# The rounded-off parts of four weight blocks made by an adding DMA and ScalarE instead of VectorE

## What is computed

```python
def _attn_ref(q, k, v, alpha):                 # per batch, head and step t
    state = alpha[t] * state + outer(k[t], v[t])
    y[t] = q[t] @ state
def _moe_ref(x, w_val, conv_w, w_out):
    gate = sigmoid(causal 5-tap convolution of x per feature)
    return (gate * (x @ w_val)) @ w_out
def _moe2_ref(x, w_ch1, w_ch2):
    u = x + real(fft(fft(x, axis=1), axis=2))
    un = (u - mean(u)) / np.sqrt(var(u) + 1e-06)
    return u + np.maximum(un @ w_ch1, 0.0) @ w_ch2
```

## Time and profile before

| | us |
|---|---|
| median of 3 runs | 550.87 |
| lowest, highest | 550.78, 551.3 |
| the profiled execution | 550.92 |
| its span in the trace | 548.8 |

### The profile page before, as it was taken

How to read it: one execution, slowest core, us unless ns; L and a number is a source line. 1 busy time by engine, 2 the same in 40 slices (tenths; PEclk the granted TensorE clock), 3 DMA queues, 4 the chain that set the end, 5 groups by cost and what they waited for, 6 DMA issues and landing times.

```text
span 548.8 us, 13477 instructions
## 1 busy us (share of the span) xinstructions
PE 540.8 (99%) x5547; PEld 519.5 (95%) x5547; DVE 400.5 (73%) x898; ACT 208.3 (38%) x487; POOL 13.0 (2%) x29
## 2 busy tenths in 40 slices
PE   7999999999999999999999999999999999999997
PEld 6988999999999999999999999999999999999997
DVE  7999899989858686989767486998936484653322
ACT  5565454425352135335262144325244133322221
POOL 0010000000000000000000000000000000000000
PEclk9999999999999999999999999999999999999999
DMA  8778202354312010455322001256300000022000
GB/s 255 237 265 301 67 25 63 112 159 133 82 47 81 30 33 26 136 145 175 93 62 68 29 1 45 85 142 191 83 4 27 30 2 0 1 59 83 11 23 30
DMA packets 36300, 47.20 MB, mean 86 GB/s; under 512 B 11632, under 2 KB 25200, under 8 KB 35984
## 3 DMA queue, kind: packets, MB, share of 16 engines
q1 hardware_dynamic: 34080, 40.97, 24.8%
q0 software_dynamic: 1728, 5.11, 2.6%
q10 hardware_dynamic: 432, 0.27, 0.2%
HBM read 35.32 MB, written 11.01 MB: 84 GB/s over the span
## 4 chain that ended last, share of the span: by engine, by line
PE 92%; DVE 4%; issue 1%; DMA 1%; ACT 1%; SPq 0%; DVEq 0%
PE bank L1062 45%; PE bank L1151 28%; PE evens L1089 4%; PE bank L1136 4%; PE bank L1131 2%; PE bank L1219 2%; PE bank L1182 2%; PE sums L1113 2%; PE bank L1253 1%; PE bank L1188 1%; DMA k_in<-in_k_dram 1%; DVE w_lo L985 1%; PE bank L1263 1%; PE sums L1098 0%; DVE scores L947 0%
## 5 line engine op out<-in xcount | busy, mean ns | idle before, releaser
L1044 DVE SCALAR_TENSOR_TENSOR h_lo<-bank,h_hi 128x256 fp32r<-128x256 f32 x144 | 60.2, 419 | 93.7 <-ACT h_hi L786 89.2
L1062 PE MATMUL bank<-unT_hi,w_hi 128*128 128x256 f32 x432 | 123.8, 286 | 1.0 <-DVE h_lo L1044 0.7
L786 ACT ACTIVATE h_hi<-bank 128x256 fp32r<-128x256 f32 x144 | 55.2, 383 | 177.0 <-PE bank L1062 176.9
L1062 PE MATMUL bank<-unT_lo,w_hi 128*128 128x256 f32 x432 | 122.1, 283 | 0.0
L1062 PE MATMUL bank<-unT_hi,w_lo 128*128 128x256 f32 x432 | 121.3, 281 | 0.0
L1151 PE MATMUL bank<-w_hi,h_hi 128*128 128x384 f32 x288 | 98.8, 343 | 0.0
L1151 PE MATMUL bank<-w_lo,h_hi 128*128 128x384 f32 x288 | 97.6, 339 | 0.0
L1151 PE MATMUL bank<-w_hi,h_lo 128*128 128x384 f32 x288 | 97.3, 338 | 0.0
L1062 PEld LDWEIGHTS bank<-unT_hi,w_hi 128*128 128x128 f32 x432 | 81.2, 188 | 4.3 <-DVE h_lo L1044 2.0
L1062 PEld LDWEIGHTS bank<-unT_hi,w_lo 128*128 128x128 f32 x432 | 81.6, 189 | 0.0
L1062 PEld LDWEIGHTS bank<-unT_lo,w_hi 128*128 128x128 f32 x432 | 81.4, 189 | 0.0
(11 more groups left out here) (192 smaller groups left out, 1016.5 us busy)
## 6 DMA issues: line engine op xcount, KB each, us to landing
v_in<-in_v_dram SPq DMA_DIRECT2D x24, 224.0 KB, 2.9
w_raw<-in_w_dram SPq DMA_DIRECT2D x2, 2304.0 KB, 10.3
a_in<-in_alpha_dram SPq DMA_DIRECT2D x44, 96.9 KB, 2.3
q_in<-in_q_dram SPq DMA_DIRECT2D x44, 96.0 KB, 2.2
k_in<-in_k_dram SPq DMA_DIRECT2D x44, 96.0 KB, 2.3
turned_blocks<-turned SPq DMA_DIRECT2D x15, 256.0 KB, 2.2
kdT<-turned_blocks SPq DMA_DIRECT2D x60, 64.0 KB, 2.0
out_dram<-u POOLq DMA_DIRECT2D x18, 192.0 KB, 2.4
```

The source lines that it names most:

```text
L786: act.activation(h_hi[:, f % HBUF, :], ps[:, 0:GW], ACT.Relu).then_inc(s_hi, 1)
L1044: dve.scalar_tensor_tensor(h_lo[:, f % HBUF, :], ps[:, 0:GW], 0.0, h_hi[:, f % HBUF, :].bitcast(F32), ALU.max, ALU.subtract).then_inc(s_re ...
L1062: last = pe.matmul(ps, l, r, start=(i == 0), stop=(i == len(mms) - 1))
```

## The change

Pieces 1 and 2 of `w1` and `w2` (four blocks) are prepared another way; piece 0 and all other tables are not touched. For each of the four blocks:

1. ACT's `whi` writes minus the rounded weights (scale -1) to the place of the high part.
2. POOL waits for it and issues a DMA from that place to the raw weights, with addition (`accum_op`): in the raw weights' bytes now stands raw minus high. It moves 128 x 1536 elements of 4 bytes, 768 KB, from SBUF to SBUF. A semaphore of its own tells its end.
3. ACT's new form of `wlo` waits for that semaphore and writes the sum onto itself, rounded to fp32r. DVE's subtraction is gone.
4. ACT's new step `wpos` multiplies the high part by -1 in place. PE waits for this step (`weights_hi_positive`) instead of DVE's.

The steps are placed anew: `whi` of both pieces 1 moves from the MLP's slots 0 and 1 to the front, right behind `whi` of `w2`'s piece 0; the new `wlo` of `w1` piece 1 stands at the front's end, ahead of the steps `t`; the others are listed in `FIRST`.

```diff
@@ front(b)
-        sch += [("wlo", 0, WN.index("w1"), 0)] + attention(n, 0, "inv") + [("whi", 0, WN.index("w2"), 0)]
+        sch += [("wlo", 0, WN.index("w1"), 0)] + attention(n, 0, "inv") + [("whi", 0, WN.index("w2"), 0), ("whi", 0, WN.index("w1"), 1), ("whi", 0, WN.index("w2"), 1)]
...
-        sch += attention(n, 0, "scale")
+        sch += attention(n, 0, "scale") + [("wlo", 0, WN.index("w1"), 1)]
@@ FIRST
-         "wlo": ((1, 1, "w1"), (2, 1, "w2"), (6, 2, "w1"), (7, 2, "w2")), "x": (15, 26), "gate": (25, 36),
+         "wlo": ((0, "wpos", "w1", 1), (1, "wlo", "w2", 1), (2, "wpos", "w2", 1), (2, "whi", "w1", 2), (3, "whi", "w2", 2), (6, "wlo", "w1", 2), (6, "wpos", "w1", 2), (7, "wlo", "w2", 2), (8, "wpos", "w2", 2)), "x": (15, 26), "gate": (25, 36),
@@ GpSimd
+                if kind == "whi" and by_dma(a, f):
+                    pool.wait_ge(s_whi, WHI_AT[w] + 1)
+                    raw, negative = (part(w_[WN[a]], a, f) for w_ in (w_raw, w_hi))
+                    pool.dma_start(raw, negative.bitcast(F32), accum_op=ALU.add).then_inc(s_wadd[WADD_AT[("wlo",) + w[1:]]], 16)
@@ ScalarE
-                    act.activation(high, raw, ACT.Copy, scale=0.5 if WN[a] == "wout" else 1.0).then_inc(s_whi, 1)
+                    scale = 0.5 if WN[a] == "wout" else -1.0 if by_dma(a, f) else 1.0
+                    act.activation(high, raw, ACT.Copy, scale=scale).then_inc(s_whi, 1)
+                elif kind == "wlo" and by_dma(a, f):
+                    act.wait_ge(s_wadd[WADD_AT[w]], 16)
+                    high, low, sums_ = (part(w_[WN[a]], a, f) for w_ in (w_hi, w_lo, w_raw))
+                    act.activation(low, sums_, ACT.Copy)
+                elif kind == "wpos":
+                    high = part(w_hi[WN[a]], a, f)
+                    act.activation(high, high.bitcast(F32), ACT.Copy, scale=-1.0).then_inc(s_wpos, 1)
@@ VectorE
-                elif kind == "wlo":
+                elif kind == "wlo" and not by_dma(a, f):
@@ TensorE
-                pe.wait_ge(s_wlo, WLO_AT["wlo", 0, WN.index(name), j] + 1)
+                w = ("wlo", 0, WN.index(name), j)
+                if w in WADD_AT:
+                    pe.wait_ge(s_wpos, WADD_AT[w] + 1)
+                else:
+                    pe.wait_ge(s_wlo, WLO_AT[w] + 1)
```

More of the change, by code:

```diff
@@ L108, in front @@
     if b == 0:
-        sch += [("wlo", 0, WN.index("w1"), 0)] + attention(n, 0, "inv") + [("whi", 0, WN.index("w2"), 0)]
+        sch += [("wlo", 0, WN.index("w1"), 0)] + attention(n, 0, "inv") + [("whi", 0, WN.index("w2"), 0), ("whi", 0, WN.index("w1"), 1), ("whi", 0, WN.index("w2"), 1)]
     sch += [("pq", b, 0, 0), ("pair", b, 0, 0), ("zdif", b, 1, 0), ("zsum", b, 1, 0), ("stat", b, 0, 0), ("dev", b, 0, 0)]
+    if b == 0:
+        sch += []
     sch += [("inverse", b, 0, 0), ("norm", b, 0, 0), ("norm", b, 1, 0), ("pqe", b, 0, 0), ("pqo", b, 0, 0)]
@@ L143, in mlp @@
                     slots[plan["inv"][c]] += attention(*at, "inv")
-        for a, j, name in plan["wlo"]:
-            slots[a - 1] += [("whi", 0, WN.index(name), j)]
-            slots[a] += [("wlo", 0, WN.index(name), j)]
+        for s, kind, name, j in plan["wlo"]:
+            slots[s] += [(kind, 0, WN.index(name), j)]
     for m in (1, 2):
@@ L204, with by_dma @@
 assert len(set(SCHEDULE)) == len(SCHEDULE)
+def by_dma(j, i):
+    return WN[j] in ("w1", "w2") and i > 0
 UNIT_KINDS = ("val", "v", "zdif", "u", "zsum", "oddrow", "pq", "pqe", "pqo", "t", "h", "out", "tapj", "wd", "wdl")
@@ L227 @@
     DREAD_AT["pqe", b_, 0, 0] = DREAD_AT["pqo", b_, 0, 0]
-WHI_AT, WLO_AT = order_of("whi"), order_of("wlo")
+WHI_AT = order_of("whi")
+WLO_AT = {w: j for j, w in enumerate(w for w in order_of("wlo") if not by_dma(*w[2:]))}
+WADD_AT = {w: j for j, w in enumerate(w for w in order_of("wlo") if by_dma(*w[2:]))}
 KEYS_AT, ROWS_AT = order_of("kx"), order_of("ux")
@@ L443, in build @@
         s_wlo = sem("weights_lo")
+        s_wadd = [sem(f"weights_lo_{WN[w[2]]}_{w[3]}") for w in WADD_AT]
+        s_wpos = sem("weights_hi_positive")
         s_in = [sem("qk_loaded_even"), sem("qk_loaded_odd")]
@@ L629, in _ @@
                 kind, b, a, f = w
-                if kind == "out" and b < B - 1:
+                if kind == "whi" and by_dma(a, f):
+                    pool.wait_ge(s_whi, WHI_AT[w] + 1)
+                    raw, negative = (part(w_[WN[a]], a, f) for w_ in (w_raw, w_hi))
+                    pool.dma_start(raw, negative.bitcast(F32), accum_op=ALU.add).then_inc(s_wadd[WADD_AT[("wlo",) + w[1:]]], 16)
+                elif kind == "out" and b < B - 1:
                     t = a * TG + f
```

## The result

| | us |
|---|---|
| before, median of 12 runs | 550.9 (550.0 to 551.45) |
| changed, median of 12 runs | 552.32 (551.9 to 554.48) |
| ratio, 95% interval | 1.0032, 1.0025 to 1.004 |
| the profiled execution of the changed kernel, its span | 554.28, 552.2 |

The changed kernel is 0.3% slower, 1.4 us by the medians, where the forecast had it 0.4 us faster at 550.5; the time lies inside the forecast's range, 549.8 to 553.5. Two of its 12 executions took over 554 us, the profiled one among them. A second measurement (e12) had a ratio of 1.0048 (1.0032 to 1.0064), with three of six executions of that kind.

The account below looks back on a forecast made before the run. PE was taken to bound the kernel, so only its waits pay: 0.73 lost at `h` 0, 0.92 gained at `h` 4 and 0.23 at `h` 10 give -0.42, from 550.92 to 550.5 us; range 549.8 to 553.5.

Parts of the forecast that it names:

- PE's two waits for `h_lo`: First MLP, `h` 4 and `h` 10: DVE's subtractions cost PE 0.92 + 0.23 = 1.15 us, the most to gain.
- the `wlo` ahead of `h` 0: ACT's added conversion of `w1` piece 1 delays `unT_hi`, so `h` 0 starts at 82.15, 0.73 us later.
- Free by my value: `w2` piece 2's add lands at 100.4, ACT asks at about 100.8: no wait; 2.3 us late at the upper end.
- I take the middle, 6.2 us: Time of one 768 KB add, between bounds 4.6 and 7.9 us, chosen because the queue is quiet here.
- the upper end: An add costs as twice the bytes, 1536 KB: 7.9 us, 0.7 us late for `w1` piece 1.
- the prediction's lower end: An add costs as a plain 768 KB transfer, 4.6 us; 2.6 us of it transfer, 2 us latency.
- Rival A: Late adds hold up ACT ahead of `unT_hi` and `h_hi` 8: up to +2.6 us, 553.5 us; chance 0.26.
- until ~101.6: Latest start of ACT's last `wlo`, `w2` piece 2, so that `h_lo` 8 still ends by 105.3 for `h` 10.
- Rival B: ACT is the next bound: later `h_hi` 3, 7 and 8 return the gain, about 551.1 us; chance 0.12.
- C's condition: ACT's first `wlo` hides before `h` 0, so its price isn't paid: full 1.15 us gained, 549.8 us; chance 0.04.
- ACT's idle names the adding DMA ahead of a `wlo`: Sign on ACT that the forecast is wrong: it waits for an add before converting a block.
- PE's list names `h_lo` for more than 0.3 us: Sign in the first MLP that the forecast is wrong: PE still waits for DVE's `h_lo`.

Follow-up runs that it names:

- e12: The changed kernel measured once more, word for word: 553.43 us, ratio 1.0048.
- e10: Against the changed kernel: adds for piece 1 alone, asked for behind `h_hi` 0 and `h_hi` 2, piece 2 subtracted by DVE; 550.24 us, ratio 0.9989.
- e13: e10 with two one-column memsets more on DVE at the start, into a tile nothing reads; 549.35 us, ratio 0.9974.
- e1: Changed kernel without the four adding DMAs and ACT's waits for them, all ACT steps kept; 550.52 us, ratio 1.0002.
- e2: Changed kernel with adds for piece 1 alone, piece 2 subtracted by DVE as before; 551.37 us, ratio 1.0006.
- e4: Changed kernel with plain copies of the same bytes in place of the adds, same issues and waits; 550.55 us, ratio 0.9995.
- e6: Changed kernel with ACT asking for the last add behind `h_hi` 8 instead of ahead of it; 552.97 us, ratio 1.0043.
- e9: Changed kernel without adds or waits for them; four plain 768 KB stores to an unused buffer at piece 2's time; 552.48 us, ratio 1.0025.
- e5: Changed kernel with piece 2's `whi` steps two slots earlier, so its adds leave earlier; 552.28 us, ratio 1.0028.
- e8: Changed kernel with `wlo` of `w1` piece 1 behind `h_hi` 0 and piece 2's `whi` in slots 1 and 2; 552.24 us, ratio 1.0043.
- e7: Changed kernel with three adds, `w2` piece 2 subtracted by DVE with its `whi` in slot 6; 552.4 us, ratio 1.0029.

## Why the prediction was wrong

**Right: what bounds the kernel, and what is to be had.** PE's two waits for `h_lo` were priced at 1.15 us. The wait of `h` 4 went away as told (`h` 4 at 89.75 with none; 89.88 was forecast), and e10 and e13 took 1.08 and 1.14 of it to `h_lo` 71.

**Right in kind, 0.11 short: the `wlo` ahead of `h` 0.** It ran without idle from 78.91, and `h` 0 began 0.84 us later than before against the first `V_lo` (81.99 - 63.46 and 81.42 - 63.73), where 0.73 was forecast. The terms on ACT behind it held too: where the DMAs make no one wait (e1, e2, e4), `h_lo` 71 comes 0.26 to 0.27 us earlier, against -0.42, of which 0.11 is this.

**The step that failed: the DMA of `w2` piece 2, "Free by my value".** Its first part was mis-sized. For a single add "I take the middle, 6.2 us" was near (6.5 to 7.2), and for piece 1 ACT never waited. For the second of a pair the sum reckoned 4.2 us of transfer behind the first; it took 6.7 (landings at 96.7 and 103.4), so that it landed at 103.4 and not at 100.4. Two things were in it. The addition itself was priced nearly right: an add held the engines for 4.4 us (e4), 4.6 in the pair of piece 2 (0.76 of 12 us for two), where the middle value had 4.2 of transfer and the upper end 5.9. The kind of cost named for the upper end, "it must read both addends, so it may cost as twice the bytes", is borne out, as the same bytes cost 2.1 times a copy's DMA time; but a copy took 2.1 us of the engines and not the 2.6 of the prediction's lower end. The Trainium skill, "Collectives: The Full Stack", The bandwidth ceiling, which the prediction named, has half a copy's rate for an adding transfer in a collective; this case's ratio of 2.1 agrees with it. What was left out is that the 16 engines are shared. The reason for the middle, a quiet queue, looked at the adds' own queue and at the DMA share of 80 to 92 us, 0.26; from 92 to 104 it was 0.32 in the kernel before, 3.8 us of all engines, and SP's transfers still took 0.28 beside the adds, 3.4 us. By these shares two adds and SP's transfers together need 12.5 us of the engines in that stretch of 12 (an estimate), which is why the second landed at 103.4. The upper end had 103.8, near the mark partly by luck, with a dearer add and no sharing. Rival A at its upper end had 2.3 us for this place; ACT waited 1.98.

**The part that no term held: the other transfers.** Free "until ~101.6" was reckoned for ACT alone. The prediction asked who waits for the adds and not who waits for transfers beside them. `lam` on DVE, which waited 2.96 us for an `alpha` load, and the state sums on PE, whose turned keys came late through SP's queue, lose nearly as much as ACT's wait does: where ACT asks later the sums start as late (e6, 1.05 us at `h` 10 and 0.99 at the sums), and where nobody waits for the transfers that fill the engines 1.8 us are lost (e9). Moving the adds earlier shifts the loss to the turned keys (e5, e8). Rival A named one mechanism in two places; two more, as dear, stood in neither.

**The sum put right.** -0.42 + 0.11 + 1.98 of ACT's wait at the last place = +1.7. The trace has `h` 10 1.62 us later than before (106.96 - 63.46 against 105.61 - 63.73) and the state sums 1.94, so 550.92 + 1.6 to 1.9 = 552.5 to 552.9 us; the executions with full clock took 551.9 to 553.0. In the others the clock falls after the wait: `h_lo` 8 is 1.62 us late and `h_lo` 11 is 3.58, so 1.96 us more is lost between 107 and 112 us, 0.3 of it at the sums, and 552.3 becomes 554.3. Rival B stayed small in the changed kernel, since `h_hi` 3 to 7 came in time. C's condition (the first price not paid) did not occur, but e10 reached the same by asking later.

**The signs.** "ACT's idle names the adding DMA ahead of a `wlo`" and "PE's list names `h_lo` for more than 0.3 us" were named as what would make the forecast wrong, and both came.

## What to carry to other kernels

Taking work off an engine by a DMA is priced by three questions: how long the transfer takes from issue to landing, when its consumer asks, and which small loads with less slack than that are issued while it runs. The third decided here: a 97 KB load that had come in 2.1 to 3.2 us came in 8.0 to 9.5. What stands behind it in the issuing engine's queue leaves late as well, as the turned keys did here. Early in the front, where no load is urgent, the same adds were free and the change pays, if the wait for them stands behind what PE waits for next (e13, 1.5 us faster by the medians, 1.14 of it seen up to `h_lo` 71). And before a 0.1% result is put down to an edit, see whether stretches that the edit doesn't reach kept their length; two idle instructions moved this kernel by 0.7 us.

## What the runs showed of the hardware

- An adding DMA between places of SBUF (768 KB, 128 partitions): 7.0 us alone (e7), 6.5 to 7.2 as the first of a pair, and 8.3 to 11.6 as the second, issued up to 3.3 us behind; a copy of the same bytes 4.3 to 5.9 (e4). An add takes 4.4 us of all 16 engines, a copy 2.1. POOL's issue takes 0.88 to 1.3 us instead of 0.56 to 0.76.
- DMA engines at a share of 1.04 (208 GB/s in all, 0.76 of the share for adds) delay a 97 KB load to 8.0 to 9.5 us; beside a pair of adds in e8 a 64 KB load took up to 9.4. Plain stores at 0.95 and 346 GB/s do nearly the same (5.6 to 8.4). SP's issues stretch as well: the two of the `alpha` loads took 1.61 us instead of 0.79, two `k` loads 3.15 instead of 0.89.
- TensorE's granted clock fell (0.50 from 109 to 112 us) after a stretch in which PE was busy 2.36 of 4 us. Executions of this program with a mean clock of 0.997 were 2 of 12 and 3 of 6, and took some 2 us more. e5, e6, e7 and e8 had waits of the same length or longer (e8: PE busy 1.44 of 4 us) and a clock of 1.00 throughout in their traces; among the executions without a trace, one of e6 and two of e8 had a lower clock. What tells them apart stays open.
- From the end of ACT's `h_hi` to the start of DVE's `h_lo`, with DVE idle, it took 0.10 us in the kernel before, and 0.48 at the same place with two DVE instructions fewer ahead.
